# Attention sums copied unscaled and turned one group later, rows scaled by VectorE and tokens by dims by GpSimd, and the first gather two groups sooner

## What is computed

```python
# attention, 8 heads of 64; n_global = 8, n_local = 96
scores = scale * q @ k.T - slope[h] * dist          # masked to the window and the first keys
a = exp(scores - max);  a = a / (sum(a) + 1e-9)
x = a @ v                                            # (batch, token, 512)
# mixing over tokens of rank 32, and a feed-forward layer
u = x + (x.transpose @ U @ V).transpose
u = u + relu(u @ w_ch1) @ w_ch2
# a gated layer
h = relu(u @ w_in); a, b = halves of h; b = normalise(b)
out = (a * (w_spatial @ b + b_spatial)) @ w_out
```

## Time and profile before

| what | value |
|---|---|
| median of 3 runs | 499.96 us (499.73 to 501.85) |
| the profiled execution | 499.4 us |
| its span, first to last instruction | 497.4 us |
| PE busy | 483.4 us, 97% |
| PEld, DVE, ACT, POOL busy | 403.8, 308.4, 224.5, 251.4 us |
| granted TensorE clock | 1.00 throughout |
| attention, until `hidden(0)` begins | 0 to 96.63 us |

### The profile page before, as it was taken

One profiled execution on the slowest core, in us unless ns is written; L12 is line 12 of the kernel. 1 busy time (PEld: TensorE's weight loads), 2 busy tenths in 40 slices (PEclk: granted clock), 3 DMA queues, 4 the chain that ended last, 5 costly groups with the idle time before them and its releaser, 6 DMA issues.

```text
span 497.4 us, 7981 instructions
## 1 busy us (share of the span) xinstructions
PE 483.4 (97%) x2756; PEld 403.8 (81%) x2756; DVE 308.4 (62%) x731; ACT 224.5 (45%) x519; POOL 251.4 (51%) x222
## 2 busy tenths in 40 slices
PE   8889899799999999999999999999999999999997
PEld 8678578587888888888888888888888888998986
DVE  6878679421259455564565646557878888888600
ACT  7889879542235543341332413315352356333122
POOL 6978666454335776735586456231886200950000
DMA  5565643232222420222130120220212000001022
GB/s 177 177 184 164 191 144 86 78 126 86 85 84 86 169 86 5 81 84 85 50 120 20 66 86 1 86 63 0 65 63 82 36 1 1 2 0 43 21 86 105
DMA packets 19113, 39.48 MB, mean 79 GB/s; under 512 B 3840, under 2 KB 7168, under 8 KB 19072
## 3 DMA queue, kind: packets, MB, share of 16 engines
q1 hardware_dynamic: 17056, 35.55, 21.7%
...
...
## 4 chain that ended last, share of the span: by engine, by line
PE 68%; DVE 8%; POOL 8%; DMA 5%; ACT 4%; issue 3%; SPq 3%; DVEq 2%; POOLq 0%; ACTq 0%
PE bank L1885 15%; PE bank L1819 9%; PE bank L1743 9%; PE bank L1967 8%; PE bank L1914 8%; PE bank L1907 8%; PE bank L1610 7%; DMA inv_rows<-inv_scratch 2%; SPq L428 2%; DMA inv_scratch<-inv_T 2%; ACT prob L1265 1%; POOL sp_op L650 1%; PE bank L1668 1%; DVEq L1094 1%; POOL qk_split L544 1%
## 5 line engine op out<-in xcount | busy, mean ns | idle before, releaser
L595 POOL TENSOR_TENSOR w_slot<-stage,w_slot 128x1024 fp32r<-128x1024 f32 x30 | 73.3, 2453 | 65.7 <-ACT w_slot L1341 65.7
L1026 DVE TENSOR_TENSOR uT<-bank,uT 128x512 f32<-128x512 f32 x68 | 45.8, 690 | 25.3 <-PE bank L1914 23.2
L1265 ACT ACTIVATE prob<-prob,row_min 128x256 f32<-128x256 f32 (+1 forms) x96 | 46.2, 483 | 3.9 <-DVE row_min L822 3.4
L1885 PE MATMUL bank<-u_op,s_slot 128*128 128x512 f32 x192 | 47.6, 389 | 0.0
L1819 PE MATMUL bank<-hid,w_slot 128*128 128x512 f32 x192 | 46.9, 393 | 0.0
L1743 PE MATMUL bank<-u_split,w_slot 128*128 128x512 f32 x192 | 46.4, 391 | 0.0
L1907 PE MATMUL bank<-hid,w_slot 128*128 128x512 f32 x192 | 46.1, 389 | 0.0
L1914 PE MATMUL bank<-hid,w_slot 128*128 128x512 f32 x192 | 46.1, 389 | 0.0
L1064 DVE TENSOR_TENSOR part<-part,bank 128x512 f32<-128x512 f32 x40 | 27.5, 686 | 26.9 <-PE bank L1885 26.5
L1819 PEld LDWEIGHTS bank<-hid,w_slot 128*128 128x128 f32 x192 | 35.7, 188 | 8.2 <-issue 0.9
L1885 PEld LDWEIGHTS bank<-u_op,s_slot 128*128 128x128 f32 x192 | 36.0, 188 | 7.5
...
## 6 DMA issues: line engine op xcount, KB each, us to landing
...
```

What stands on the lines that cost most here:

```text
L595: nc.gpsimd.tensor_tensor(dst[:, LO, :], stage[n % 2][:, 0:w], dst[:, HI, :].bitcast(F32), ALU.subtract).then_inc(w_lo, 1)
L1026: vec.tensor_tensor(y, y_bank(e)[:], y, ALU.add).then_inc(y_sum, 1)
L1265: last = sc.activation(prob[r][:, e, 0:w], prob[r][:, e, 0:w], ACT.Exp, bias=row_min[:, k:k + 1], scale=-1.0, accum_out=row_sum[:, q:q + 1])
L1885: last = mm(seven_bank[held][:], lhs, u_op[op][:, m, k, :], start=not more and k == 0 and p == 0, stop=k == 1 and p == 2, skip_group_check ...
```

## The change

- `copy_o` copies the unscaled sums of every group to uT on VectorE, in its round s for group s, so the copy needs no table. `turn_x(s - 1)` stands in TensorE's round s, where `turn_x(s - 2)` stood.
- `take_x` is VectorE's, for all groups: it multiplies the turned sums in PSUM by the inverses of the rows and writes `x_all`. ScalarE doesn't do it any more.
- `scale_u(g)` on GpSimd multiplies the tokens by dims of every group in place by the table; it stands in GpSimd's iteration g + 2, ahead of `split_qk(g + 4)`, and frees the table buffer.
- 1e-9 is added by VectorE, from a tile `eps` in SBUF, in `invert`; `add_eps` is gone from ScalarE.
- ScalarE copies both halves of `probT` from group 2 on; VectorE both for groups 0 and 1.
- VectorE transposes the inverses after the second half of its scores, not before the first scale.
- `GATHER` is 12, `MIX_AT` (14, 16, 18, 20); `sum_u` waits for `x_late`; `turn_x(23)` follows `hidden(0)`.

```diff
-        GATHER = 14
-        MIX_AT = (16, 18, 20, 20)
+        GATHER = 12
+        MIX_AT = (14, 16, 18, 20)
...
                 sp.wait_ge(inv_out[g % 2], 16 * (g // 2 + 1))
-                if g == 3:
-                    sp.wait_ge(x_late, 1)
-                elif g > 3:
-                    sp.wait_ge(xT_sb, g - 2)
+                if g >= 3:
+                    sp.wait_ge(x_late, g - 2)
...
-            def scale_late():
-
-                pool.wait_ge(inv_in[0], 32)
-                pool.wait_ge(x_ps, 1)
-                nc.gpsimd.tensor_tensor(x_tile(0), x_tile(0), inv_rows[0][:], ALU.mult).then_inc(x_late, 1)
+            def scale_u(g):
+
+                pool.wait_ge(inv_in[g % 3], 32 * (g // 3 + 1))
+                pool.wait_ge(x_ps, g + 1)
+                nc.gpsimd.tensor_tensor(x_tile(g), x_tile(g), inv_rows[g % 3][:], ALU.mult).then_inc(x_late, 1)
...
+                    if g >= 2:
+                        scale_u(g - 2)
                     if 6 <= g + 4 < QUADS:
                         split_qk(g + 4)
-                    if g == 1:
-                        scale_late()
...
+                scale_u(QUADS - 2)
+                scale_u(QUADS - 1)
...
             def take_probT(g):
                 w = 2 * P * blocks(g // 2)
-                if g < 2:
-
-                    dve.wait_ge(turned, 2 * g + 1)
-                    vec.tensor_copy(probT[2 * g][:, 0:w], pt_bank[0][:, 0:w]).then_inc(probT_a, 1)
+                dve.wait_ge(turned, 2 * g + 1)
+                vec.tensor_copy(probT[2 * g][:, 0:w], pt_bank[0][:, 0:w]).then_inc(probT_0, 1)
                 dve.wait_ge(turned, 2 * g + 2)
-                if g >= 2:
-                    dve.wait_ge(pv_done, g - 1)
-                vec.tensor_copy(probT[(2 * g + 1) % 4][:, 0:w], pt_bank[1][:, 0:w]).then_inc(probT_d, 1)
+                vec.tensor_copy(probT[2 * g + 1][:, 0:w], pt_bank[1][:, 0:w]).then_inc(probT_1, 1)
 
             def invert(g):
                 q = slice(g % 4 * 4, g % 4 * 4 + 4)
+                if g == 0:
+                    dve.wait_ge(inv_set, 4)
+                dve.wait_ge(expd, 2 * g + 2)
+                vec.tensor_tensor(row_one[:, q], row_sum[:, q], eps[:], ALU.add).then_inc(sum_eps, 1)
                 dve.wait_ge(sum_eps, g + 1)
-                if g == 0:
-                    dve.wait_ge(inv_set, 3)
                 if g >= 3:
                     dve.wait_ge(inv_turned, g - 2)
-                if g == 3:
-                    dve.wait_ge(x_half, 1)
+                    dve.wait_ge(x_half, g - 2)
...
-            def copy_o():
-
-                dve.wait_ge(pv_done, 1)
-                vec.tensor_copy(x_tile(0), x_bank(0)[:, 0:256].rearrange("p (c q) -> p c q", c=2)).then_inc(xT_sb, 1)
-
...
+            def copy_o(g):
+
+                dve.wait_ge(pv_done, g + 1)
+                vec.tensor_copy(x_tile(g), x_bank(g)[:, 0:256].rearrange("p (c q) -> p c q", c=2)).then_inc(xT_sb, 1)
+
+            def take_x(g):
+
+                t, hq = divmod(g, 2)
+                dve.wait_ge(x_ps, g + 1)
+                if t == XS and hq == 0:
+                    dve.wait_ge(z_acc, 1)
+                vec.tensor_tensor(x_all[:, t % XS, hq * 256:hq * 256 + 256].rearrange("p (m e d) -> p m e d", m=2, e=2),
+                                  x_bank(g)[:, 0:256].rearrange("p (m e d) -> p m e d", m=2, e=2),
+                                  row_inv[g % 3][:, :, 0].rearrange("p (e m) -> p m e", e=2).unsqueeze(3).to_broadcast([P, 2, 2, D]),
                                   ALU.mult).then_inc(x_half, 1)
-
-            def scale_x(g):
-
-                dve.wait_ge(inv_in[g % 3], 32 * (g // 3 + 1))
-                dve.wait_ge(pv_done, g + 1)
-                vec.tensor_tensor(x_tile(g), x_bank(g)[:, 0:256].rearrange("p (c q) -> p c q", c=2),
-                                  inv_rows[g % 3][:], ALU.mult).then_inc(xT_sb, 1)
...
+                dve.wait_ge(x_late, (8, 12, 16, 24)[j // KD])
...
-                for s in range(-2, QUADS + 1):
+                for s in range(-2, QUADS):
                     if s + 2 < QUADS:
                         score_bias(s + 2, 0)
                         if s < 1:
                             score_bias(s + 2, 1)
-                    if 0 <= s + 1 < QUADS:
-                        if s < 1:
-                            take_probT(s + 1)
-                        invert(s + 1)
-                        turn_inverse(s + 1)
-                    if s == QUADS - 2:
-                        take_probT(s + 1)
-                    if s == 1:
-                        copy_o()
-                    if s >= 2:
-                        scale_x(s - 1)
-                    if s == 15:
-                        split_z(0)
-                    if s == MIX_AT[0]:
-                        dve.wait_ge(x_late, 1)
                     for j in range(FIRST):
                         if s == MIX_AT[j]:
                             sum_u(j)
-                    if s >= 1:
-                        if s + 2 < QUADS:
-                            score_bias(s + 2, 1)
-                        if s + 1 < QUADS - 1:
-                            take_probT(s + 1)
-                        if s == 1:
-                            take_x0()
+                    if s in (-1, 0):
+                        take_probT(s + 1)
+                    if 0 <= s + 1 < QUADS:
+                        invert(s + 1)
+                    if s >= 0:
+                        copy_o(s)
+                    if s == GATHER + 1:
+                        split_z(0)
+                    if s >= 1 and s + 2 < QUADS:
+                        score_bias(s + 2, 1)
+                    if 0 <= s + 1 < QUADS:
+                        turn_inverse(s + 1)
+                    if s >= 0:
+                        take_x(s)
...
+                act.wait_ge(pv_done, g - 1)
                 act.wait_ge(turned, 2 * g + 1)
-                act.wait_ge(pv_done, g - 1)
-                sc.activation(probT[2 * g % 4][:, 0:w], pt_bank[0][:, 0:w], ACT.Copy).then_inc(probT_a, 1)
-
-            def add_eps(g):
...
-            def take_x(g):
...
+                sc.activation(probT[2 * g % 4][:, 0:w], pt_bank[0][:, 0:w], ACT.Copy).then_inc(probT_0, 1)
+                act.wait_ge(turned, 2 * g + 2)
+                sc.activation(probT[2 * g % 4 + 1][:, 0:w], pt_bank[1][:, 0:w], ACT.Copy).then_inc(probT_1, 1)
...
                     if s >= 1:
                         take_probT(s + 1)
-                        if s >= 2:
-                            take_x(s - 1)
                     if 1 <= s and g < QUADS and s != GATHER:
                         exps(g, 1)
-                        add_eps(g)
...
-                if f == 0:
-                    take_x(QUADS - 2)
-                if f == 1:
-                    take_x(QUADS - 1)
...
-                if g in (19, 21):
-
-                    pe.wait_ge(u_sum, (g - 17) // 2)
-                if g == 23:
-                    pe.wait_ge(u_sum, FIRST)
+                if g in (17, 19, 21, 23):
+
+                    pe.wait_ge(u_sum, (g - 15) // 2)
...
-                    if s >= 2:
-                        turn_x(s - 2)
+                    if s >= 1:
+                        turn_x(s - 1)
...
                     hidden(f)
                 if f == 1:
                     pe.wait_ge(u_sum, FIRST)
-                    turn_x(QUADS - 1)
                 if f == 2:
                     pe.wait_ge(x_half, QUADS)
                     mix(4)

```

34 lines of the change are left out of this document (9 added, 25 removed).

## The result

The changed kernel took 507.59 us (median of 4 runs, 506.63 to 509.35), the kernel before beside it 500.9. The ratio is 1.0138, with a 95% interval from 1.0096 to 1.0179: 1.4% slower, clear of the noise, and above the 505.5 us at which the range ended. The forecast started from 499.96 us, so 0.9 us of what it missed is scatter of the kernel before. A second comparison, in a later set of runs, gave 1.0132 (1.0104 to 1.0159). The profiled execution of the changed kernel took 509.35 us with a span of 507.3, the slowest of the four, and that of the kernel before took 499.4, 1.5 us under its median here.

What follows compares the result with a forecast made beforehand. TensorE's own work was taken to bound rounds without waits, and GpSimd, left without air, to set the result. Terms of +0.4 - 1.6 + 3.8 - 1.4 + 0.6 + 0 = +1.8 on 499.96 gave 501.8 us, range 496.3 to 505.5.

Steps and rivals of the forecast that it cites:

- a forecast of 3.8: Rounds 8 and 9: GpSimd's iterations with split_V come late and hold up TensorE, +3.8 us.
- the one foreseen for round 19: Round 19: a wait of weigh for copy_v of about 2 us, as a sign that the forecast is right.
- Rounds 0 to 3, +0.4: Start of the attention: TensorE stands in round 1 for copy_o(0), partly offset by holes that go, +0.4 us.
- two small holes: Rounds 0 to 3: said to disappear along with that of round 3, in exchange for the stand in round 1.
- Round 6: The 1.60 us hole before the turn of the sums goes, as copy_o needs only weigh: -1.6 us, called sure.
- nothing left: Round 7: copy_v(7) would be ready at 35 us, just when weigh(7) wants it, with no time in hand.
- Rounds 15 to 22, +0.6: GpSimd's iterations with half a weight stage and split_u make TensorE wait: 30.2 us against 29.6 now, +0.6.
- less than 2: Iterations 16 to 18: GpSimd's lead in us to meet its 4.7 us excess over TensorE, leaving a 3.0 us wait.
- From T(23) on, 0: From the turn of group 23 to hidden(2): later transpose of inverses and freer store queue cancel, 0 us.
- VectorE behind GpSimd: Rival: VectorE's addition of eps waits for GpSimd's instruction, 2.9 us over 24 rounds, 504.7 us or more; chance 0.31.
- The rival's 504.7 us: Time if VectorE's addition of eps waits for GpSimd's instruction under way, met at random over 24 rounds; chance 0.31.

Runs made afterwards that it cites:

- the first comparison: Changed kernel without VectorE's addition of 1e-9, first time, ratio against the kernel before: 502.88 us, 1.0069; the changed kernel had taken 507.59 us.

## Why the prediction was wrong

The frame held: GpSimd is the engine that sets the result up to T(23), rounds 4 to 6 are at 3.17 us, and rounds 8 and 9 took 5.29 and 5.20 us, 3.95 more up to T(12) against a forecast of 3.8. The holes stand at `weigh` in rounds 8 and 17 (1.92 and 2.27 us); in round 9 only 0.39 us is a wait, since TensorE is slow there at the low clock, and the one foreseen for round 19 is missing in this profile and 1.98 us long in that of the later set. Without the multiplication the kernel is even with the one before. The sum failed at these steps; two of them, rounds 15 to 22 and the end, make 6.3 of the 8.1 us between the rows and the sum.

- **Rounds 0 to 3, +0.4.** Measured +1.44: "two small holes" were one of 2.00 us, with the clock down behind it. The size was wrong, and it didn't matter, as T(8) shows.
- **Round 6, "-1.6. This is sure".** This is the step that failed in its reasoning, worth 1.3 us at T(8) (+0.07 measured, -1.2 in the sum). The wait for table 4 was taken off VectorE, but the table didn't come sooner: GpSimd waited 1.28 for it at 32.72, and `copy_v(7)` stood behind. I had worked out all of that two paragraphs on ("nothing left") and still booked the gain. Counted from a T(4) on time, the hole comes back as one of 1.8 to 2.4 ahead of `weigh(7)`. So T(8) stays, and the true sum up to T(12) is 0 + 4.0 and not 0.4 - 1.6 + 3.8.
- **Rounds 15 to 22, +0.6.** Measured +3.80, the largest miss. I gave GpSimd "less than 2" us of lead in hand there; table 13 landed 2.20 us after GpSimd was ready for it, and the lead was gone. The wait of 2.27 at `weigh(17)` was then near the 3.0 forecast in size, but with 1.6 of clock behind it, and the rest had 0.49 for `copy_o(18)`, 1.11 at `weigh(21)` and 1.38 for `copy_o(21)`, where I had 1.0 and 0.7. The waits are 5.25 against 4.7, so the term was short mostly by what it had no entry for: the clock, and the addition held behind GpSimd. Each of the three mixes also takes some 0.45 us from start to start and not 0.3. GpSimd's iteration of 3.4 us was a little too long: it is 3.17.
- **From T(23) on, 0.** I set the later transpose (0.6) against a freer queue (0.4 to 0.6). Measured +1.40 and +1.72 of clock. The load was issued 5.73 us behind T(23) and not 4.45 (5.2 to 6.2 in every changed version with the late load): +1.28. It took 5.41 to its use and not 4.90: +0.51. The air of 0.39 met that much of it. The queue isn't freer: the transpose of group 22, behind the copy and the scores now, comes 0.85 us ahead of T(23) (98.25) where it came 3.31 ahead (88.82), and its store, its spread and the store of group 23 follow it one by one. No run moved the transpose alone, so its share is read from the rows. The whole chain with its clock is some 2 us of the median, by the runs with the load early.
- **The clock, no term at all.** In the earlier trace rows a hole of 1.60 us left the clock up, and I didn't ask what a longer one would do. By the run with idle products it is some 1.5 to 2 us, of which the drop at `hidden(2)` is in the previous step too.
- **VectorE behind GpSimd, kept out of the forecast.** Right in mechanism, at 2.42 us for one addition. In time it is 1.3 us at T(23), and at the end between nothing and 1.3 in the later set; how much of the first comparison's 3.5 to 4.7 us was luck in load and clock stays open.

The rival's 504.7 us was nearer, but mostly not for its reason: of its 2.9 us the rows show 1.3 at T(23), and the losses behind T(23) and those of the clock were in neither sum.
